# Attention and two MLPs on one core: batch 1's gate and value tiles computed as products of 2x2 blocks

## The chip, the cores and the metric

The kernel is one program on one core of a Trainium2 chip. The metric is the time of the program on the device in microseconds; the median of the runs counts. TensorE (PE in the rows) multiplies, ScalarE (ACT) and VectorE (DVE) read its results from the eight PSUM banks, GpSimd (POOL) works in SBUF, and SyncE (SP) issues DMAs. Each engine works through its own queue in order, and semaphores are all that ties one queue to another.

## The reference

Windowed attention with block summaries (batch 2, 8 heads, 768 tokens, width 64) gives x of 1536 tokens by 512. Two MLPs follow, and the change touches only the first, and of that only batch 1:

```
rms = sqrt(mean(x*x) + 1e-6);  xn = x / rms * rms_g
g   = xn @ w_gate              # 512 x 1536
val = xn @ w_val               # 512 x 1536
y   = (g * sigmoid(g) * val) @ w_out      # 1536 x 512
h   = y @ w_in                 # 512 x 2048
out = (h - tanh(h)) @ w_out2   # 2048 x 512
```

## The kernel before

Every fp32 matrix is held as two fp32r parts, high (a rounded copy, made by ScalarE) and low (the remainder, a subtraction on VectorE), and each product of fp32 matrices is three matmuls: high by high, high by low, low by high. Inputs of the MLPs lie transposed: `xT_hi[g]` and `xT_lo[g]` hold batch g's x^T as 4 chunks of 128 rows by 768 tokens. Tokens are worked in halves of 384 (NB), so that a result fits a bank.

The order of the work is written out by hand for each engine. Batch 0's attention comes first; batch 1's attention is woven into batch 0's first MLP. Then come batch 0's projection down (`down_first`, tiles z), batch 0's second MLP, batch 1's first MLP (gates and values, then `down_first`), and batch 1's second MLP.

In the first MLP the 1536 columns of `w_gate` and `w_val` make 12 row tiles j of 128 (J1). For each j and token half b, `gate` and `val` make 4 chunks x 3 = 12 matmuls each (through `project`) into banks `XB` and `YB`. ScalarE takes the tanh, VectorE makes `sg` and `pd` (`gated`, `product`), ScalarE makes the high part of h and VectorE the low part (`low_h`). Tiles of weights come by DMA into `x_raw` (gate) and `y_raw` (value), two slots each, are split into `x_hi`, `x_lo`, `y_hi`, `y_lo`, and are used for two halves.

The second MLP already multiplies by seven instead of eight (Winograd's form of Strassen's scheme). A pair p of row tiles and the two token halves make a 2x2 block matrix; `quarter` is one block product, 2 chunks x 3 = 6 matmuls of 128 x 384. GpSimd makes sums of the weights' blocks (`add_weights`: four adds of 128x256 into `ws_raw`), which ScalarE and VectorE split. Sums accumulate in one bank, and ScalarE keeps the intermediate states (`keep_part`). Between the quarters of pair p stand the 12 output units (`down_unit`, 3 matmuls of 128 x 512) of pair p-1. That covers the waits between quarters. In the trace the second MLP's tiles `h2_hi` and `h2_lo` are named `h_hi` and `h_lo`.

## Time and profile before

| | us |
|---|---|
| median of 3 runs (645.47 to 649.68) | 645.63 |
| the profiled execution, as a run | 643.8 |
| its span, first to last instruction | 642.1 |
| TensorE busy | 625.2 (97%) |
| VectorE busy | 386.6 (60%) |
| ScalarE busy | 293.8 (46%) |
| GpSimd busy | 122.5 (19%) |

The span is divided by the order of work. By first instructions on TensorE, batch 0's second MLP ends at 362.59 us, batch 1's gates and values at 462.45 us, and its projection down at 512.37 us. Matmuls are pipelined, so that the time that one costs is the distance from its start to the next one's start, not its printed duration. The granted TensorE clock is 1.00 in every stretch, which is the higher of its two levels, 2.4 GHz.

### The profile page before, as it was taken

To read this page: it belongs to the slowest core of one execution; us is meant where nothing else is said; L and a number is where in the kernel's file an instruction comes from. 1 tells how busy PE (TensorE), PEld (TensorE's weight loads), DVE (VectorE), ACT (ScalarE), POOL (GpSimd) and SP (SyncE) were. 2 spreads that over 40 slices of the span, in tenths; PEclk is the share of its full clock that TensorE was granted. 3 is DMA by queue.
4 is the path that set the end of the run, shared out by engine and by line. 5 is a ranking of instruction groups with operands and counts; after the bars stand their busy time and mean duration, and the time that the engine had idled before them with its cause. 6 is when DMAs were issued, how large, how long until landed. Compare 5 with 4: busy or idle time off the path is not lost.

```text
span 642.1 us, 10665 instructions
## 1 busy us (share of the span) xinstructions
PE 625.2 (97%) x4086; PEld 583.5 (91%) x4086; DVE 386.6 (60%) x647; ACT 293.8 (46%) x564; POOL 122.5 (19%) x175
## 2 busy tenths in 40 slices
PE   8888999999999999999999999999999999999997
PEld 7567889999999998988899899999999989998886
DVE  3787667666653569766664455555433398666643
ACT  4685454454533347555554333333233275555532
POOL 3674612021210222222220000000100033222200
PEclk9999999999999999999999999999999999999999
DMA  9994913321412123222212422111313013222102
GB/s 260 211 207 126 200 50 91 91 58 34 102 40 74 51 91 84 80 66 67 65 50 66 148 66 63 53 54 47 99 50 114 2 51 99 76 71 66 35 1 98
DMA packets 96170, 53.91 MB, mean 84 GB/s; under 512 B 33720, under 2 KB 90296, under 8 KB 95928
## 3 DMA queue, kind: packets, MB, share of 16 engines
q1 hardware_dynamic: 94824, 50.87, 30.7%
q10 hardware_dynamic: 1296, 2.36, 1.0%
q8 instruction: 33, 0.54, 0.4%
q14 instruction: 17, 0.14, 0.1%
HBM read 50.07 MB, written 3.15 MB: 83 GB/s over the span
## 4 chain that ended last, share of the span: by engine, by line
PE 87%; SPq 5%; ACT 3%; DVE 3%; issue 1%; DMA 1%; POOL 0%; DVEq 0%; POOLq 0%; ACTq 0%
PE bank L726 14%; PE bank L728 14%; PE bank L727 14%; PE bank L834 7%; PE bank L833 7%; PE bank L832 7%; PE bank L786 6%; PE bank L788 6%; PE bank L790 6%; SPq L384 3%; PE bank L710 1%; PE bank L586 1%; PE bank L690 1%; PE bank L661 1%; ACT kT L1010 1%
## 5 line engine op out<-in xcount | busy, mean ns | idle before, releaser
L1412 DVE TENSOR_TENSOR h_lo<-pd,h_hi 128x384 fp32r<-128x384 f32 x112 | 67.2, 601 | 38.9 <-ACT h_hi L1090 24.5
L834 PE MATMUL bank<-y_hi,h_lo 128*128 128x512 f32 x192 | 75.5, 393 | 0.0
L833 PE MATMUL bank<-y_lo,h_hi 128*128 128x512 f32 x192 | 75.4, 393 | 0.0
L832 PE MATMUL bank<-y_hi,h_hi 128*128 128x512 f32 x192 | 75.3, 392 | 0.0
L572 POOL TENSOR_TENSOR ws_raw<-x_raw 128x256 f32<-128x256 f32 x16 | 12.2, 760 | 325.4 <-DMA x_raw<-in_moe_w_in_dram 146.3
L726 PE MATMUL bank<-xT_hi,x_hi 128*128 128x384 f32 x192 | 65.1, 339 | 1.4 <-DVE xT_lo L1408 1.4
L726 PE MATMUL bank<-xT_hi,y_hi 128*128 128x384 f32 x192 | 65.7, 342 | 0.0
L726 PE MATMUL bank<-h_hi,z_hi 128*128 128x384 f32 x192 | 64.9, 338 | 0.0
L728 PE MATMUL bank<-h_hi,z_lo 128*128 128x384 f32 x192 | 64.5, 336 | 0.0
L727 PE MATMUL bank<-h_lo,z_hi 128*128 128x384 f32 x192 | 64.5, 336 | 0.0
L728 PE MATMUL bank<-xT_hi,y_lo 128*128 128x384 f32 x192 | 64.3, 335 | 0.0
L728 PE MATMUL bank<-xT_hi,x_lo 128*128 128x384 f32 x192 | 64.2, 335 | 0.0
L727 PE MATMUL bank<-xT_lo,y_hi 128*128 128x384 f32 x192 | 64.2, 334 | 0.0
L727 PE MATMUL bank<-xT_lo,x_hi 128*128 128x384 f32 x192 | 64.2, 334 | 0.0
L1090 ACT CAST h_hi<-pd 128x384 fp32r<-128x384 f32 x48 | 24.7, 514 | 85.8 <-DVE pd L1440 85.7
L1440 DVE SCALAR_TENSOR_TENSOR pd<-sg,bank 128x384 f32<-128x384 f32 x48 | 26.6, 553 | 39.3 <-PE bank L728 38.9
L1493 DVE TENSOR_TENSOR total<-part,bank 128x384 f32<-128x384 f32 x48 | 26.4, 553 | 34.8 <-ACT part L1123 28.9
L1123 ACT COPY part<-bank 128x384 f32<-128x384 f32 x48 | 23.0, 479 | 52.0 <-PE bank L790 50.8
L834 PEld LDWEIGHTS bank<-y_hi,h_lo 128*128 128x128 f32 x192 | 36.0, 188 | 8.2
L1412 DVE TENSOR_TENSOR y_lo<-y_raw,y_hi 128x512 fp32r<-128x512 f32 x56 | 40.2, 722 | 0.1
L833 PEld LDWEIGHTS bank<-y_lo,h_hi 128*128 128x128 f32 x192 | 36.0, 188 | 4.0
L1133 ACT ACTIVATE th<-total 128x384 f32<-128x384 f32 x48 | 25.2, 525 | 31.5 <-DVE total L1493 31.5
(141 smaller groups left out, 1457.3 us busy)
## 6 DMA issues: line engine op xcount, KB each, us to landing
x_raw<-in_moe_w_in_dram SPq DMA_DIRECT2D x32, 256.0 KB, 3.3
y_raw<-in_moe_w_out_dram SPq DMA_DIRECT2D x32, 256.0 KB, 2.7
x_raw<-in_moe_w_gate_dram SPq DMA_DIRECT2D x24, 256.0 KB, 3.2
y_raw<-in_moe_w_val_dram SPq DMA_DIRECT2D x24, 256.0 KB, 3.3
z_raw<-in_moe_w_out_dram SPq DMA_DIRECT2D x16, 384.0 KB, 3.4
k_rows<-in_k_dram SPq DMA_DIRECT2D x8, 384.0 KB, 6.1
qn<-in_q_dram SPq DMA_DIRECT2D x12, 256.0 KB, 6.7
vw_early<-in_v_dram SPq DMA_DIRECT2D x12, 192.0 KB, 6.1
```

Of the source, the lines that this page charges most:

```text
L726: nc.tensor.matmul(dst, w_hi, a_hi, start=start, stop=False)
L727: nc.tensor.matmul(dst, w_hi, a_lo, start=False, stop=False)
L728: return nc.tensor.matmul(dst, w_lo, a_hi, start=False, stop=stop)
L786: nc.tensor.matmul(dst, w_hi[:, r, :], a_hi[:, r, :], start=start and r == 0, stop=False, skip_group_check=True)
L788: nc.tensor.matmul(dst, w_hi[:, r, :], a_lo[:, r, :], start=False, stop=False, skip_group_check=True)
L790: last = nc.tensor.matmul(dst, w_lo[:, r, :], a_hi[:, r, :], start=False, stop=r == 1, skip_group_check=True)
L832: nc.tensor.matmul(AB[t][:], a_hi, w_hi, start=begins, stop=False, skip_group_check=True)
L833: nc.tensor.matmul(AB[t][:], a_hi, w_lo, start=False, stop=False, skip_group_check=True)
L834: last = nc.tensor.matmul(AB[t][:], a_lo, w_hi, start=False, stop=ends, skip_group_check=True)
L1412: nc.vector.tensor_tensor(dst, full, high.bitcast(f32), ALU.subtract).then_inc(done, 1)
L1440: nc.vector.scalar_tensor_tensor(out=pd[:, s, :], in0=sg[:, s, :], scalar=0.5, in1=YB[vpos % 2][:, 0:NB], op0=ALU.mult, op1=ALU.mult).then ...
L1493: nc.vector.tensor_tensor(total[:, TOTALS.index(name[:3]), :], kept, accumulator, ALU.add).then_inc(total_done, 1)
```

## The change

- Batch 1's gates and values are made pair by pair (6 pairs i of row tiles, 2i and 2i+1) by the same scheme of seven block products. Each is done for gate and value in turn (`up_pair` in all engines): P1, P2, P5, P6, P7, P4, P3, 14 `quarter` calls of 6 matmuls for a pair. Before, a pair was 8 calls of `project` with 12 matmuls.
- Nothing stands between the quarters of a pair on TensorE. P2 accumulates on a copy of P1 that ScalarE writes into another bank (`keep_up`). P6, P7 and P4 accumulate on P1 in place, with copies of the state after P6 (`kept2`) and P7 (`kept3`). VectorE joins P5 to them, one join directly into the bank in which P3 then accumulates.
- GpSimd forms the sums of the weights' blocks in eight adds of 128x256 per pair (`add_up_weights`), for the next pair while TensorE works on this one. ScalarE and VectorE split them (`us_hi`, `us_lo`; 1024 elements for the gates, the same for the values, which ScalarE does in two instructions of 512). The second row tile of a pair is split only in its lower half (256 elements).
- The sums of batch 1's x^T (`x_sums`) are formed during pairs 1 to 7 of batch 0's second MLP: 14 VectorE instructions of 128x768, two in each pair, and 4 ScalarE copies of 128x768. They stand behind the pair's `split_sums`.
- At the end of batch 0 the six output stores move from ScalarE's queue to SP's, which issues them behind the loads of the second pair of gate and value tiles. ScalarE and VectorE split the first sums between their copies of output rows. The first two z tiles of batch 1 are split in the last pair of gates and values, and no longer in batch 0.

The diff, cut to the products, the sums and the orders of the engines:

```diff
+        UP_ORDER = [(name, m) for name in ("P1", "P2", "P5", "P6", "P7", "P4", "P3") for m in (GATE, VAL)]
+        UP_TILES = ("C11", "C22", "C21", "C12")
+        KEPT = [("P1", GATE), ("P1", VAL), ("P6", GATE), ("P6", VAL), ("P7", GATE), ("P7", VAL)]
...
+            def add_up_weights(i):
+                if i < 2:
+                    pool.wait_ge(quarter_mm, PRODUCTS * NP)
+                else:
+                    pool.wait_ge(block_mm, len(UP_ORDER) * (i - 1))
+                for m in (GATE, VAL):
+                    raw, landed, at = (x_raw, x_in, 8 * i) if m == GATE else (y_raw, y_in, 8 * i + 4)
+                    for row in range(2):
+                        pool.wait_ge(landed[row], (up_weight(i, row) - row) * 8 + 16)
+                    s = [us_raw[i % 2][:, m, k, :, :] for k in range(4)]
+                    a11, a12, a21, a22 = (raw[:, row, c:c + KH, :] for row in range(2) for c in (0, KH))
+                    nc.gpsimd.tensor_tensor(s[S1], a21, a22, ALU.add).then_inc(us_added, 1)
+                    nc.gpsimd.tensor_tensor(s[S3], a11, a21, ALU.subtract).then_inc(us_added, 1)
+                    pool.wait_ge(us_added, at + 1)
+                    nc.gpsimd.tensor_tensor(s[S2], s[S1], a11, ALU.subtract).then_inc(us_added, 1)
+                    pool.wait_ge(us_added, at + 3)
+                    nc.gpsimd.tensor_tensor(s[S4], a12, s[S2], ALU.subtract).then_inc(us_added, 1)
...
+                return {"P1": lambda: weights(0, top) + x(top, first),
+                        "P2": lambda: weights(0, bottom) + x(bottom, first),
+                        "P3": lambda: sums(S4) + x(bottom, rest),
+                        "P4": lambda: weights(1, bottom) + x_sums(T4),
+                        "P5": lambda: sums(S1) + x(top, rest),
+                        "P6": lambda: sums(S2) + x_sums(T2),
+                        "P7": lambda: sums(S3) + x_sums(T3)}[name]()
+            def up_pair(i):
+                def product(name, m, dst, start=False):
+                    quarter(dst, *up_operands(i, name, m), start=start).then_inc(block_mm, 1)
+                if i == 0:
+                    pe.wait_ge(ts_dve, 14)
+                for m in (GATE, VAL):
+                    pe.wait_ge(y_lo_done if m else x_lo_done, up_weight(i, 0) + 1)
+                    if i:
+                        pe.wait_ge(c22_done, 2 * (i - 1) + m + 1)
+                    elif m:
+                        pe.wait_ge(out_act, 1)
+                    product("P1", m, sum_bank(i, m), start=True)
+                for m in (GATE, VAL):
+                    pe.wait_ge(kept_done, kept_no(i, "P1", m))
+                    product("P2", m, c11_bank(m))
+                for m in (GATE, VAL):
+                    pe.wait_ge(us_lo_done, 2 * i + m + 1)
+                    if i:
+                        pe.wait_ge(prod_done if m else x_bank_free, up_pos(i - 1, "C21") + 1)
+                    elif m:
+                        pe.wait_ge(out_dve, 1)
+                    product("P5", m, p5_bank(i, m), start=True)
+                for m in (GATE, VAL):
+                    product("P6", m, sum_bank(i, m))
+                for m in (GATE, VAL):
+                    pe.wait_ge(kept_done, kept_no(i, "P6", m))
+                    product("P7", m, sum_bank(i, m))
+                for m in (GATE, VAL):
+                    pe.wait_ge(y_lo_done if m else x_lo_done, up_weight(i, 1) + 1)
+                    pe.wait_ge(kept_done, kept_no(i, "P7", m))
+                    product("P4", m, sum_bank(i, m))
+                for m in (GATE, VAL):
+                    pe.wait_ge(joined, 2 * i + m + 1)
+                    product("P3", m, c12_bank(m))
...
+            def split_up_sums(i, m, part=slice(0, 4)):
+                act.wait_ge(us_added, 8 * i + 4 * m + 4 if part.stop == 4 else 8 * i + 4 * m + 3)
+                nc.scalar.copy(us_hi[i % 2][:, m, part, :, :], us_raw[i % 2][:, m, part, :, :]).then_inc(us_hi_done, 1)
...
+            def up_pair(i):
+                if i:
+                    tanh_up(i - 1, "C12")
+                    high_up(i - 1, "C21")
+                keep_up(i, "P1", GATE)
+                if i + 1 < J1 // 2:
+                    split_x(up_weight(i + 1, 0))
+                keep_up(i, "P1", VAL)
+                if i:
+                    high_up(i - 1, "C12")
+                tanh_up(i, "C11")
+                if i + 1 < J1 // 2:
+                    split_y(up_weight(i + 1, 0))
+                    split_x(up_weight(i + 1, 1))
+                    split_y(up_weight(i + 1, 1))
+                else:
+                    split_z(ZG)
+                    split_z(ZG + 1)
+                if i + 1 < J1 // 2:
+                    split_up_sums(i + 1, GATE)
+                    split_up_sums(i + 1, VAL, slice(S1, S3))
+                high_up(i, "C11")
+                keep_up(i, "P6", GATE)
+                if i + 1 < J1 // 2:
+                    split_up_sums(i + 1, VAL, slice(S3, 4))
+                keep_up(i, "P6", VAL)
+                keep_up(i, "P7", GATE)
+                keep_up(i, "P7", VAL)
+                tanh_up(i, "C22")
+                tanh_up(i, "C21")
+                high_up(i, "C22")
...
+            def x_sums(i):
+                hi11, hi21 = (xT_hi[1][:, c:c + KH, 0:NB].bitcast(f32) for c in (0, KH))
+                lo11, lo21 = (xT_lo[1][:, c:c + KH, 0:NB].bitcast(f32) for c in (0, KH))
+                hi12, hi22 = (xT_hi[1][:, c:c + KH, NB:S].bitcast(f32) for c in (0, KH))
+                lo12, lo22 = (xT_lo[1][:, c:c + KH, NB:S].bitcast(f32) for c in (0, KH))
+                t1 = kT[1][:, 0:KH, NB:S]
+                t2, t3, t4 = (ts_raw[:, k, :, :] for k in (T2, T3, T4))
+                dve.wait_ge(ts_dve, 2 * (i - 1))
+                if i == 1:
+                    dve.wait_ge(z_mm, ZG)
+                    dve.wait_ge(xT_lo_done, NT)
+                    nc.vector.tensor_tensor(ts_raw_hi[:, T3, :, :], hi22, hi12, ALU.subtract).then_inc(ts_dve, 1)
+                    nc.vector.tensor_tensor(t3, lo22, lo12, ALU.subtract).then_inc(ts_dve, 1)
...
+                if i == 4:
+                    nc.vector.tensor_tensor(t1, t2, t4, ALU.add).then_inc(ts_dve, 1)
+                    dve.wait_ge(ts_dve, 7)
+                    nc.vector.tensor_tensor(t2, hi22, t1, ALU.subtract).then_inc(ts_dve, 1)
+                if i == 5:
+                    nc.vector.tensor_tensor(t2, t2, lo22, ALU.add).then_inc(ts_dve, 1)
+                    dve.wait_ge(ts_act, 2)
+                    low(xT_lo[1][:, 0:KH, NB:S], t1, xT_hi[1][:, 0:KH, NB:S], ts_dve)
...
+            def join(i, m):
+                dve.wait_ge(kept_done, kept_no(i, "P6", m))
+                dve.wait_ge(block_mm, block_no(i, "P5", m))
+                if i:
+                    dve.wait_ge(prod_done if m else x_bank_free, up_pos(i - 1, "C12") + 1)
+                else:
+                    dve.wait_ge(out_dve, 2 + m)
+                nc.vector.tensor_tensor(c12_bank(m), kept2[:, m, :], p5_bank(i, m), ALU.add).then_inc(joined, 1)
+            def join_c22(i, m):
+                dve.wait_ge(kept_done, kept_no(i, "P7", m))
+                nc.vector.tensor_tensor(kept3[:, m, :], kept3[:, m, :], p5_bank(i, m), ALU.add).then_inc(c22_done, 1)
...
+            def up_pair(i):
+                last = i + 1 == J1 // 2
+                if i:
+                    gated_up(i - 1, "C12")
+                    low_up(i - 1, "C21")
+                    product_up(i - 1, "C12")
+                if not last:
+                    split_x(up_weight(i + 1, 0))
+                if i:
+                    low_up(i - 1, "C12")
+                if not last:
+                    split_y(up_weight(i + 1, 0))
+                gated_up(i, "C11")
+                if not last:
+                    split_x(up_weight(i + 1, 1))
+                product_up(i, "C11")
+                if not last:
+                    split_y(up_weight(i + 1, 1))
+                else:
+                    split_z(ZG)
+                    split_z(ZG + 1)
+                low_up(i, "C11")
+                if not last:
+                    split_up_sums(i + 1, GATE)
+                join(i, GATE)
+                join(i, VAL)
+                join_c22(i, GATE)
+                join_c22(i, VAL)
+                gated_up(i, "C22")
+                product_up(i, "C22")
+                gated_up(i, "C21")
+                low_up(i, "C22")
+                product_up(i, "C21")
+                if not last:
+                    split_up_sums(i + 1, VAL)
```

What stands on an engine now, at three places. GpSimd, batch 0's last weight sums and what follows them; before, these rows go straight to batch 1's second MLP:

```order
L572 TENSOR_TENSOR ws_raw0<-x_raw 128x256
L573 TENSOR_TENSOR ws_raw0<-x_raw 128x256
L575 TENSOR_TENSOR ws_raw0<-ws_raw0,x_raw 128x256
L577 TENSOR_TENSOR ws_raw0<-x_raw,ws_raw0 128x256
L572 TENSOR_TENSOR ws_raw1<-x_raw 128x256
```

Of the change, in its place, a part of the 48 new adds, with numbers left off the buffers:

```order
L717 TENSOR_TENSOR us_raw<-x_raw,us_raw 128x256
L712 TENSOR_TENSOR us_raw<-y_raw 128x256
L713 TENSOR_TENSOR us_raw<-y_raw 128x256
L715 TENSOR_TENSOR us_raw<-us_raw,y_raw 128x256
L717 TENSOR_TENSOR us_raw<-y_raw,us_raw 128x256
L694 TENSOR_TENSOR ws_raw<-x_raw 128x256
```

The adds for six pairs, eight for each, now stand ahead of batch 1's `ws_raw` adds.

ScalarE, batch 1's gates and values, before (two row tiles' rows repeat like this):

```order
L1066 CAST x_hi<-x_raw 128x512
L1073 CAST y_hi<-y_raw 128x512
L1085 ACTIVATE th<-bank 128x384
L1090 CAST h_hi<-pd 128x384
L1085 ACTIVATE th<-bank 128x384
L1090 CAST h_hi<-pd 128x384
```

and now, a pair from its first tanh to its last copy of the state:

```order
L1338 ACTIVATE th<-bank 128x384
L1274 CAST y_hi2<-y_raw 128x512
L1266 CAST x_hi2<-x_raw 128x256
L1274 CAST y_hi2<-y_raw 128x256
L1310 CAST us_hi1<-us_raw1 128x1024
L1310 CAST us_hi1<-us_raw1 128x512
L1291 CAST h_hi<-pd 128x384
L1329 COPY kept2<-bank 128x384
L1310 CAST us_hi1<-us_raw1 128x512
L1329 COPY kept2<-bank 128x384
L1329 COPY kept3<-bank 128x384 x2
```

The copies of the next pair's sums, which wait for GpSimd, now stand ahead of this pair's copy of P6, for which TensorE waits before P7.

VectorE, a pair of batch 0's second MLP, before:

```order
L1412 TENSOR_TENSOR h2_lo<-pd,h2_hi 128x384
L1412 TENSOR_TENSOR ws_lo1<-ws_raw1,ws_hi1 128x1024
L1493 TENSOR_TENSOR total<-part,bank 128x384
L1502 TENSOR_TENSOR pd<-total,th 128x384
L1502 TENSOR_TENSOR pd<-bank,th 128x384
```

and now:

```order
L1697 TENSOR_TENSOR h2_lo<-pd,h2_hi 128x384
L1697 TENSOR_TENSOR ws_lo0<-ws_raw0,ws_hi0 128x1024
L1697 TENSOR_TENSOR ts_lo<-ts_raw,ts_hi 128x768
L1758 TENSOR_TENSOR ts_raw<-xT_lo1 128x768
L1892 TENSOR_TENSOR total<-part,bank 128x384
L1901 TENSOR_TENSOR pd<-total,th 128x384
```

Two instructions of 768 elements stand between the split of the weight sums and the total that the pair needs next.

## Rows read from the trace of the kernel before

**Rows 1.** The page: span, busy time of the engines, and the chain by engine.

```profile
span 642.1 us, 10665 instructions
...
PE 625.2 (97%) x4086; PEld 583.5 (91%) x4086; DVE 386.6 (60%) x647; ACT 293.8 (46%) x564; POOL 122.5 (19%) x175
...
PE 87%; SPq 5%; ACT 3%; DVE 3%; issue 1%; DMA 1%; POOL 0%; DVEq 0%; POOLq 0%; ACTq 0%
```

**Rows 2.** Busy time by stretch: window, length, PE, PEld, DVE, ACT, POOL, clock, DMA.

```profile
362.59:462.50 99.91, 99.91 (x578) 99.91 (x577) 52.97 (x93) 34.59 (x70) 3.17 (x4) 1.00 0.25 74
```

**Rows 3.** TensorE in order of time (start, us): first instructions of two stretches.

```profile
362.59 0.34 PE L726 MATMUL bank<-xT_hi,x_hi 128*128 128x384 f32 x1
...
462.45 0.33 PE L726 MATMUL bank<-h_hi,z_hi 128*128 128x384 f32 x1
```

**Rows 4.** All engines in order of time, first pair of batch 1's second MLP.

```profile
512.37 0.34 PE L786 MATMUL bank<-xT_hi,x_hi 128*128 128x384 f32 x1
...
515.88 0.34 PE L790 MATMUL bank<-tq_hi,ws_lo 128*128 128x384 f32 x1
...
516.25 0.48 ACT L1123 COPY part<-bank 128x384 f32<-128x384 f32 x1 [0.94 <-PE bank L790]
...
516.40 0.34 PE L790 MATMUL bank<-xT_hi,x_lo 128*128 128x384 f32 x1
...
516.88 0.42 PE L786 MATMUL bank<-tq_hi,ws_hi 128*128 128x384 f32 x1
```

**Rows 5.** VectorE and GpSimd in order of time, a pair of batch 0's second MLP.

```profile
321.08 0.55 DVE L1412 TENSOR_TENSOR h_lo<-pd,h_hi 128x384 fp32r<-128x384 f32 x1
...
321.98 0.74 POOL L572 TENSOR_TENSOR ws_raw<-x_raw 128x256 f32<-128x256 f32 x1 [12.11 <-PE bank L790]
...
322.39 0.75 DVE L1412 TENSOR_TENSOR h_lo<-pd,h_hi 128x384 fp32r<-128x384 f32 x1
...
322.68 1.05 POOL L573 TENSOR_TENSOR ws_raw<-x_raw 128x256 f32<-128x256 f32 x1
...
323.06 1.09 DVE L1502 TENSOR_TENSOR pd<-total,th 128x384 f32<-128x384 f32 x1
...
323.69 1.05 POOL L575 TENSOR_TENSOR ws_raw<-ws_raw,x_raw 128x256 f32<-128x256 f32 x1
...
324.82 0.74 POOL L577 TENSOR_TENSOR ws_raw<-x_raw,ws_raw 128x256 f32<-128x256 f32 x1
```

**Rows 6.** One tile's instructions, `ws_raw`: minimum, median and maximum in ns.

```profile
L573 POOL TENSOR_TENSOR ws_raw<-x_raw x16: 742/1052/1191, 217.8 to 598.7; 128x256 f32<-128x256 f32 x16
L575 POOL TENSOR_TENSOR ws_raw<-ws_raw,x_raw x16: 733/1055/1451, 218.9 to 599.7; 128x256 f32<-128x256 f32 x16
```

**Rows 7.** Groups by line and shape, 362 to 640 us (busy, mean ns | idle before).

```profile
L1412 DVE TENSOR_TENSOR ws_lo<-ws_raw,ws_hi 128x1024 fp32r<-128x1024 f32 x8 | 9.8, 1226 | 4.4 <-ACT ws_hi L1119 4.4
...
L1412 DVE TENSOR_TENSOR z_lo<-z_raw,z_hi 128x768 fp32r<-128x768 f32 x6 | 5.7, 958 | 10.1 <-ACT z_hi L1080 10.1
```

**Rows 8.** VectorE in order of time, a pair of batch 0's second MLP.

```profile
328.42 0.69 DVE L1412 TENSOR_TENSOR y_lo<-y_raw,y_hi 128x512 fp32r<-128x512 f32 x1
...
329.02 0.42 DVE L1412 TENSOR_TENSOR x_lo<-x_raw,x_hi 128x256 fp32r<-128x256 f32 x1
...
330.61 1.22 DVE L1412 TENSOR_TENSOR ws_lo<-ws_raw,ws_hi 128x1024 fp32r<-128x1024 f32 x1 [0.71 <-ACT ws_hi L1119]
...
333.86 0.56 DVE L1493 TENSOR_TENSOR total<-part,bank 128x384 f32<-128x384 f32 x1 [2.02 <-ACT part L1123]
```

**Rows 9.** ScalarE in order of time, batch 0's second MLP.

```profile
329.15 0.48 ACT L1123 COPY part<-bank 128x384 f32<-128x384 f32 x1
...
329.53 1.05 ACT L1119 CAST ws_hi<-ws_raw 128x1024 fp32r<-128x1024 f32 x1
...
333.35 0.48 ACT L1123 COPY part<-bank 128x384 f32<-128x384 f32 x1 [2.76 <-PE bank L790]
...
340.31 0.52 ACT L1139 CAST h_hi<-pd 128x384 fp32r<-128x384 f32 x1
...
340.72 0.62 ACT L1073 CAST y_hi<-y_raw 128x512 fp32r<-128x512 f32 x1
```

More of the change, by code:

```diff
@@ L238, in halves, with blocks @@
             return [(j, 0), (j, 1), (j + 1, 0), (j + 1, 1)]
+        def blocks(i):
+            return [(2 * i, 0), (2 * i + 1, 1), (2 * i + 1, 0), (2 * i, 1)]
         first_order = {(g, j, b): n for g in range(G)
-                       for n, (j, b) in enumerate(h for i in range(J1 // 2) for h in halves(g, i))}
+                       for n, (j, b) in enumerate(h for i in range(J1 // 2) for h in (blocks(i) if g else halves(g, i)))}
         def first_pos(g, j, b):
@@ L422, in _ @@
                 if g:
-                    for j in range(J1):
-                        load_xy(weight_no(g, j))
+                    for i in range(J1 // 2):
+                        for row in range(2):
+                            load_x(up_weight(i, row))
+                        for row in range(2):
+                            load_y(up_weight(i, row))
+                        if i == 1:
+                            for t in range(TT):
+                                sp.wait_ge(out_dve if t % 2 else out_act, t // 2 + 1)
+                                sp.dma_start(out_v[:, t, :], stage[:, t, :]).then_inc(out_sent, 16)
+                    for m in range(2):
+                        load_z(ZG * g + m)
                 load_pair(g * NP)
-                for m in range(2, ZG + 2 if g + 1 < G else ZG):
+                for m in range(2, ZG):
                     load_z(ZG * g + m)
@@ L816, in operands, with up_operands, weights, sums @@
                         "P7": lambda: sums(S3) + x2_sums(T3)}[name]()
+            def up_operands(i, name, m):
+                top, bottom, first, rest = slice(0, KH), slice(KH, KC), slice(0, NB), slice(NB, S)
+                w_hi, w_lo = (t[2 * (i % 2)] for t in ((xw_hi, xw_lo) if m == GATE else (yw_hi, yw_lo)))
+                def weights(row, half):
+                    return w_hi[:, row, half, :], w_lo[:, row, half, :]
+                def sums(k):
+                    return us_hi[i % 2][:, m, k, :, :], us_lo[i % 2][:, m, k, :, :]
+                def x(half, tokens):
+                    return xT_hi[1][:, half, tokens], xT_lo[1][:, half, tokens]
+                def x_sums(k):
+                    return ts_hi[:, k, :, :], ts_lo[:, k, :, :]
+                return {"P1": lambda: weights(0, top) + x(top, first),
[5 more added lines that the diff above has]
+                        "P7": lambda: sums(S3) + x_sums(T3)}[name]()
@@ L995, in _ @@
                     for i in range(J1 // 2):
-                        for j, b in halves(g, i):
-                            gate(g, j, b)
-                            val(g, j, b)
+                        up_pair(i)
                     for d in range(KC):
@@ new lines, in split_up_sums @@
+            def split_up_sums(i, m):
+                dve.wait_ge(us_hi_done, 3 * i + 2 * m + 1)
+                low(us_lo[i % 2][:, m, :, :, :], us_raw[i % 2][:, m, :, :, :], us_hi[i % 2][:, m, :, :, :], us_lo_done)
+            def join(i, m):
+                dve.wait_ge(kept_done, kept_no(i, "P6", m))
+                dve.wait_ge(block_mm, block_no(i, "P5", m))
+                if i:
+                    dve.wait_ge(prod_done if m else x_bank_free, up_pos(i - 1, "C12") + 1)
+                else:
+                    dve.wait_ge(out_dve, 2 + m)
+                nc.vector.tensor_tensor(c12_bank(m), kept2[:, m, :], p5_bank(i, m), ALU.add).then_inc(joined, 1)
```

290 lines of the change are left out of this document (230 added, 60 removed).

## The prediction

> **What bounds the kernel now.** I read the page first. TensorE is busy 97% of the span, and 87% of the chain that ended last is TensorE's own work [rows 1]. The reader should see that nothing else carries a share, so a removed matmul is worth its own time, if nothing else comes late in its place. Next I read the stretch that the change rewrites, by its window. TensorE never pauses in it, while VectorE works 52.97 us of 99.91, ScalarE 34.59 and GpSimd 3.17, all at clock 1.00 [rows 2]. The stretch runs from 362.59 to 462.45 us [rows 3] and holds 12 row tiles x 2 halves x 2 (gate, value) x 12 = 576 matmuls, so one costs 99.86 / 576 = 0.1734 us. The printed 0.34 us overlaps with the next one. Third, I looked for a place where quarters stand on TensorE with nothing between them, as all of them will in this stretch: the first pair of batch 1's second MLP [rows 4]. Last, I looked at what VectorE and GpSimd do to each other when both work [rows 5], since both are loaded much more.
>
> **What is removed.** Six pairs x 14 quarters x 6 matmuls = 504 take the place of 576. The order of the changed program has 72 fewer TensorE rows, so the saving in number is sure. In price, 504 x 0.1734 = 87.4 us at the rate of the old stretch. Among quarters the rate is a little lower: from 512.37 to 516.40 stand 24 matmuls, 23 distances, 0.175 each [rows 4]. That place is the nearer one, so I take 504 x 0.175 = 88.2, a gain of 99.9 - 88.2 = 11.7 us before any wait, and 12.5 as the best case. A pair then takes TensorE 14.7 us, a quarter 1.05.
>
> **What each engine has to do in 14.7 us.** From start to start, VectorE takes 0.60 for 512 elements [rows 8]. By the same gap of 0.09 under the printed time, it takes 0.47 for 384, 0.33 for 256 and 1.14 for 1024 [rows 5, 7, 8]. A pair has 16 instructions of 384 (four each of sg, pd and low parts, four joins), two of 512, two of 256 and two of 1024: 7.5 + 1.2 + 0.7 + 2.3 = 11.7 us. ScalarE takes 0.41 for a cast or tanh of 384, 0.38 for a copy out of a bank, and by the same gap of 0.1 it takes 0.52 for 512 [rows 9]. Eight, six and four of these (512 elements, twice for weights and twice for sums), two of 256 (0.3) and one of 1024 (0.95) make 9.2 us. GpSimd has eight adds, 0.74 each at best and 0.70 from start to start [rows 5]: 5.7 us. Each fits, VectorE by the least, so the question is the order and not the sum.
>
> **Copies between quarters.** P2 waits for ScalarE's copy of P1, P7 for that of P6, P4 for that of P7. The price of this wait stands in the trace. P6's last matmul starts at 515.88, the copy at 516.25, and P7, which waits for it, at 516.88, 1.00 us after [rows 4]. In the change one quarter of the other matrix stands between, so the next matmul is due 7 x 0.175 = 1.22 us after. The wait is covered by 0.2 us, if ScalarE is free at that moment. The copy of P1 goes from bank to bank, and the join writes a bank; no row shows either. I take the 0.48 of the copy out of a bank [rows 9], since the source is the same. At 0.3 us more it would cost 0.1 us for each of six pairs, 0.6 in all. It could also be shorter, which gains nothing, as TensorE then is not waiting. The Trainium skill ("ScalarE: Activation LUTs", Step-by-step: what each stage is for) says that ScalarE's way to PSUM is faster than its way to SBUF; no row here shows it, and by it this term is nil.
>
> **Where ScalarE isn't free.** It handles P6's copy only behind the first 512 elements of the next pair's value sums and the high part of C11. Those sums wait for GpSimd's seventh add, and GpSimd begins when the pair before has ended, 0.2 us into the pair. So the chain that I expect to decide is: seven adds, then 0.03 + 0.52 (split) + 0.41 (high part) + 0.48 (copy) + 0.15 to TensorE = 1.6 us (0.03 and 0.15 are the gaps ahead of 516.25 and behind 516.73 [rows 4]). P7 is due at 8 x 1.05 = 8.4 us. The seventh add must therefore be done 6.8 us into the pair.
>
> Alone, seven adds take 7 x 0.70 and 0.2 for waits on one another, and end at 5.3. At the pace of a pair of the second MLP it is four adds in 3.55 and three more in 2.76 (323.69 + 1.05 - 321.98), which ends at 6.5 [rows 5]: still in time. But in that pair only two of four adds met VectorE, and each then took 1.05 in place of 0.74. What happens there is seen in the four ends. The low part that starts at 322.39 ends 0.42 after the first add's end; the second add ends 0.59 after that; VectorE's `pd` of 323.06 ends 0.42 after that, and the third add 0.59 after that. They take turns, as if one waited for the other's end. This holds for VectorE's instructions with two inputs in SBUF. In the first 7 us of a pair VectorE will have six such: the rest of a split of 1024 (0.5), two low parts (0.42 each) and splits of 512, 512 and 256 (0.56, 0.56, 0.29), 2.7 us together. Laid out in order, some 2.2 of it falls in front of an add. The seventh add then ends at 5.3 + 2.2 = 7.5, and P7 starts at 9.1 instead of 8.4. That is **0.75 us for each of pairs 1 to 4**, 3.0 us. The ends are 0 (adds at the pace of the rows) and 1.2 (all 2.7 in front) for each pair. Pair 0 escapes, since the adds for its successor can begin before batch 0's output is done, and pair 5 has no successor.
>
> The Trainium skill ("SBUF — State Buffer", Who interferes with whom) has a rule that speaks against this change. A VectorE instruction with two SBUF inputs and a GpSimd instruction that reads SBUF share a read interface, and the second to come is blocked until the first ends. By that rule, the trace agrees, with 1.05 for 0.74 and 1.09 for 0.55. Without the rule the sum would be 11.7 us gained, with it 8.7.
>
> **The sums of x^T.** 14 VectorE instructions of 768 elements at 0.96, 0.87 from start to start [rows 7], two in each of seven pairs: 1.8 us. They stand where VectorE ends at 331.83 and then waits 2.02 us for the kept P7, until 333.86 [rows 8]. They fit with 0.2 to spare, and I cost them at nothing. If that cover is gone, the total comes late; some 1.7 us of quarters and units still stand before P3 needs it. No `ws_raw` add runs at that time (the four end by 325.6 [rows 5]). ScalarE's four copies of 768, 0.84 each (halfway between 0.62 for 512 and 1.05 for 1024 [rows 9]), start when VectorE's first sum is done, near 332.8, and move the copy at 333.35 by 0.3 us. P4 is due two units later, so this is free too. The upper bound is 0.5 us in each pair, 3 us. The output stores leave ScalarE's queue; on SP's they stand ahead of the loads of pair 2, which nobody needs for 14 us. The z tiles are loaded at pair 5's start, into a place of their own, and are split 4 to 6 us into it, before P6's copy at 7.4.
>
> **The sum.** 99.9 - 88.2 - 3.0 = 8.7 us. The profiled execution took 643.8 with a span of 642.1; it becomes 635.1 with 633.4. The median of the runs stands 1.8 above the profiled one, and becomes 645.6 - 8.7 = **636.9 us**.
>
> **Rivals.**
> (a) No wait at all: GpSimd keeps the pace of the rows. The stretch is 87.4 to 88.2, the time 633.1 to 633.9. For it speaks that every engine has room; against it, VectorE at 80% instead of 53% of the stretch. Chance 0.25.
> (b) The forecast, 635.5 to 638.5. Chance 0.45.
> (c) VectorE becomes the bound. If each of the eight adds also holds VectorE up for 0.59, its 11.7 become 16.4 us, more than TensorE's 14.7, and six pairs take 98.4: 645.6 - 1.5 = 644.1. For it, `pd` at 323.06 took 1.09 in place of 0.55; against it, over half of VectorE's instructions have an input in a bank, and the second half of a pair is free of adds. Anything between (b) and this, with late batch 0 sums (up to 3 us), belongs here: 638.5 to 644.5. Chance 0.24.
> (d) Slower than before: GpSimd's chain alone. The slowest add in the trace took 1.45 [rows 6]. If all did, the seventh ends 0.2 + 10.2 = 10.4 us in, P7 starts at 12.0, 3.6 us late, and with 2.5 in pair 0 the stretch is 88.2 + 16.9 = 105.1: 650.9. It decides from 11.7 us of waits in all, 2.6 for each of the four and 1.5 in pair 0, which is a mean add of 1.3 us. Chance 0.04.
> (e) The change doesn't do what it says, for instance because a weight sum or a kept state makes TensorE wait in every quarter, with the same result as (d). Chance 0.02.
>
> **How the numbers follow.** A measurement of this kernel tells 1%, 6.5 us, from no change; that border is 639.2. (a), (b) and a third of (c) lie below: 0.78. The rest of (c) is within 1%: 0.16. Beyond 652.1 only the end of (d) and (e) lie; I leave 0.06 for them and for what I don't see. The range reaches from (a)'s lower end, 633.0, into (c), to 642.0.
>
> **What would show it.** The stretch has 504 matmuls at 0.173 to 0.176 us apart. Four waits before P7, in pairs 1 to 4, are ended by ScalarE's copy into `kept2`, of some 0.75 us. Adds of `us_raw` mean 0.9 to 1.1 us. ScalarE's second cast of `us_hi` (512) is released by GpSimd. In batch 0's second MLP TensorE doesn't pause, as before. The prediction is wrong if adds stay near 0.85 (then (a)), if TensorE waits for `us_lo`, `joined` or P1's copy, or if VectorE has no idle time left in a pair.

## The result: 635.9 us after 645.6, and the profile after

The changed kernel takes 635.88 us (median of 4 runs, 634.96 to 637.34) against 645.55 (4 runs), a ratio of 0.9845 with a 95% interval of 0.981 to 0.9881, so 1.2 to 1.9% faster. The forecast was 636.9, range 633.0 to 642.0.

The page's head and the window of the rewritten stretch, the rows that answer to [rows 1] and [rows 2] (the window's columns are length, PE, PEld, DVE, ACT, POOL, clock, DMA share, GB/s):

```profile
span 634.1 us, 10771 instructions
...
PE 615.5 (97%) x4014; PEld 571.9 (90%) x4014; DVE 425.3 (67%) x697; ACT 322.7 (51%) x622; POOL 170.2 (27%) x223
```

```profile
363.58:454.45 90.87, 88.50 (x506) 87.22 (x504) 75.33 (x127) 58.67 (x121) 38.56 (x39) 1.00 0.33 98
```

The stretch took 99.86 us [rows 3] and now takes 90.87, from TensorE's first matmul on `x_hi` at 363.58 to its first on `h_hi` and `z_hi` at 454.45. TensorE is now idle in 2.4 of these us by the profile, VectorE is busy for 75.3 of 90.9 us instead of 53.0 of 99.9, and GpSimd for 38.6 instead of 3.2. What stands behind the stretch lasts 179.65 us in both kernels (642.1 - 462.45 and 634.1 - 454.45). The stretch begins 0.99 us later. So the span's 8.0 us are 8.99 from the stretch, less 0.99 in front of it.

TensorE's waits, longest in total first:

```profile
PE bank L927 <- ACT kept L1329: 2.4, 4, 0.6
```

Four waits, at one place. TensorE in order of time around the first of them, in pair 1, which begins at 378.17:

```profile
378.17 0.33 PE L927 MATMUL bank<-xT_hi,x_hi 128*128 128x384 f32 x1
...
386.32 0.34 PE L931 MATMUL bank<-ts_hi,us_lo 128*128 128x384 f32 x1
387.24 0.44 PE L927 MATMUL bank<-ts_hi,us_hi 128*128 128x384 f32 x1 [0.59 <-ACT kept L1329]
387.52 0.34 PE L929 MATMUL bank<-ts_lo,us_hi 128*128 128x384 f32 x1
387.69 0.34 PE L931 MATMUL bank<-ts_hi,us_lo 128*128 128x384 f32 x1
```

P7 was due 0.17 after 386.32 and starts 0.92 after it, 0.75 late. The distance to the next matmul is 0.28 instead of 0.17, so that a wait costs some 0.85 in all. The others, at 402.68, 418.12 and 433.54, are alike: 4 x 0.85 = 3.4 us. The rest of the stretch, 90.87 - 3.4 = 87.5, is 504 matmuls at 0.1735. The chain that ends in the wait, GpSimd's adds first (start, us):

```profile
378.41 1.26 POOL L712 TENSOR_TENSOR us_raw<-x_raw 128x256 f32<-128x256 f32 x1 [8.10 <-PE bank L931]
379.63 1.05 POOL L713 TENSOR_TENSOR us_raw<-x_raw 128x256 f32<-128x256 f32 x1
380.64 1.18 POOL L715 TENSOR_TENSOR us_raw<-us_raw,x_raw 128x256 f32<-128x256 f32 x1
381.90 0.94 POOL L717 TENSOR_TENSOR us_raw<-x_raw,us_raw 128x256 f32<-128x256 f32 x1
382.80 1.19 POOL L712 TENSOR_TENSOR us_raw<-y_raw 128x256 f32<-128x256 f32 x1
383.95 0.92 POOL L713 TENSOR_TENSOR us_raw<-y_raw 128x256 f32<-128x256 f32 x1
384.83 0.92 POOL L715 TENSOR_TENSOR us_raw<-us_raw,y_raw 128x256 f32<-128x256 f32 x1
385.82 0.74 POOL L717 TENSOR_TENSOR us_raw<-y_raw,us_raw 128x256 f32<-128x256 f32 x1
```

and ScalarE, in the same pair:

```profile
383.00 1.05 ACT L1310 CAST us_hi<-us_raw 128x1024 fp32r<-128x1024 f32 x1
385.78 0.62 ACT L1310 CAST us_hi<-us_raw 128x512 fp32r<-128x512 f32 x1 [1.73 <-POOL us_raw L715]
386.30 0.51 ACT L1291 CAST h_hi<-pd 128x384 fp32r<-128x384 f32 x1
386.72 0.47 ACT L1329 COPY kept<-bank 128x384 f32<-128x384 f32 x1
```

The seventh add ends at 385.75, 7.6 us into the pair. ScalarE has waited 1.73 us for it, casts (385.78), makes the high part of C11 (386.30) and copies P6 (386.72, until 387.19), and P7 starts. Only the eighth add takes 0.74 us; the others take 0.92 to 1.26.

In batch 0's second MLP two short waits are new. VectorE in pair 1, with the two instructions for the sums of x^T ahead of the total, and ScalarE in pair 2, with the cast ahead of the copy of P7:

```profile
256.90 0.95 DVE L1750 TENSOR_TENSOR ts_raw_hi<-xT_hi 128x768 f32<-128x768 f32 x1
257.77 0.95 DVE L1751 TENSOR_TENSOR ts_raw<-xT_lo 128x768 f32<-128x768 f32 x1
258.64 0.55 DVE L1892 TENSOR_TENSOR total<-part,bank 128x384 f32<-128x384 f32 x1
```

```profile
271.36 0.84 ACT L1297 CAST ts_hi<-ts_raw 128x768 fp32r<-128x768 f32 x1 [2.16 <-DVE ts_raw L1753]
272.10 0.47 ACT L1407 COPY part<-bank 128x384 f32<-128x384 f32 x1
```

TensorE starts P3 at 259.24, right behind the total and 0.16 late, and P4 at 272.72, behind the copy and 0.13 late. With the longer distances that follow, they cost 0.26 and 0.21 us. These 0.47 are half of the 0.99 by which the stretch begins later. The other half is there at 183.75 us already (183.22 before), ahead of everything that was changed except the buffers' places. It isn't the change's: the kernel e4_drop72 below is the kernel before up to this stretch, and reaches it at 363.60. In the profiles below it begins anywhere from 363.58 to 366.87 (and at 368.33 in e3_one_more_add's, whose first 100 us had a mean granted clock of 0.95), so the front of the kernel varies by itself.

### The profile page after: what moved, and what is told of

Its sections match the earlier page's. It is cut to its first block, busy times and chain, and to the rows that moved or that the text cites. A ratio compares the mean times of both kernels' runs of the same rounds, so it can differ in the third digit from the quotient of the medians.

```text
span 634.1 us, 10771 instructions
## 1 busy us (share of the span) xinstructions
PE 615.5 (97%) x4014; PEld 571.9 (90%) x4014; DVE 425.3 (67%) x697; ACT 322.7 (51%) x622; POOL 170.2 (27%) x223
## 4 chain that ended last, share of the span: by engine, by line
PE 81%; POOL 5%; SPq 5%; ACT 4%; DVE 3%; issue 1%; DMA 1%; DVEq 0%; POOLq 0%; ACTq 0%
PE bank L870 9%; PE bank L927 9%; PE bank L871 9%; PE bank L872 9%; PE bank L929 9%; PE bank L931 9%; PE bank L1036 7%; PE bank L1035 7%; PE bank L1034 7%; SPq L497 3%; POOL us_raw L712 2%; PE bank L730 2%; PE bank L854 1%; POOL us_raw L715 1%; POOL us_raw L713 1%
## 5 line engine op out<-in xcount | busy, mean ns | idle before, releaser
L1697 DVE TENSOR_TENSOR h_lo<-pd,h_hi 128x384 fp32r<-128x384 f32 x112 | 70.3, 629 | 34.6 <-ACT h_hi L1291 18.9
L1034 PE MATMUL bank<-y_hi,h_hi 128*128 128x512 f32 x192 | 75.3, 392 | 0.0
L1291 ACT CAST h_hi<-pd 128x384 fp32r<-128x384 f32 x48 | 24.6, 513 | 38.8 <-DVE pd L1727 32.3
L1697 DVE TENSOR_TENSOR y_lo<-y_raw,y_hi 128x512 fp32r<-128x512 f32 (+1 forms) x56 | 40.4, 726 | 2.2 <-ACT y_hi L1274 2.1
L1901 DVE TENSOR_TENSOR pd<-total,th 128x384 f32<-128x384 f32 x48 | 33.5, 697 | 9.6 <-ACT th L1417 8.9
L1034 PEld LDWEIGHTS bank<-y_hi,h_hi 128*128 128x128 f32 x192 | 36.0, 187 | 4.0
L1423 ACT CAST h_hi<-pd 128x384 fp32r<-128x384 f32 x64 | 32.6, 512 | 12.7 <-DVE pd L1901 12.6
L606 POOL TENSOR_TENSOR sm<-sm,mx 128x480 f32<-128x480 f32 x24 | 23.7, 986 | 49.6 <-DVE mx L1666 49.6
L870 PEld LDWEIGHTS bank<-h_hi,z_hi 128*128 128x128 f32 x192 | 36.1, 188 | 0.2 <-issue 0.2
L871 PEld LDWEIGHTS bank<-h_lo,z_hi 128*128 128x128 f32 x192 | 36.1, 188 | 0.0
L872 PEld LDWEIGHTS bank<-h_hi,z_lo 128*128 128x128 f32 x192 | 36.1, 188 | 0.0
```

The lines of the kernel that those rows point to most:

```text
L870: nc.tensor.matmul(dst, w_hi, a_hi, start=start, stop=False)
L871: nc.tensor.matmul(dst, w_hi, a_lo, start=False, stop=False)
L872: return nc.tensor.matmul(dst, w_lo, a_hi, start=False, stop=stop)
L1034: nc.tensor.matmul(AB[t][:], a_hi, w_hi, start=begins, stop=False, skip_group_check=True)
L1423: nc.scalar.copy(h2_hi[:, p % NP % 2, row, b, :], pd[:, no % 2, :]).then_inc(h2_hi_done, 1)
L1697: nc.vector.tensor_tensor(dst, full, high.bitcast(f32), ALU.subtract).then_inc(done, 1)
```

## The experiments

Times are medians of each kernel's runs, ratios against runs of the kernel before in the same round of measurements. There were four rounds: the changed kernel; e1 to e4; e5 to e7; e8. The kernel before took 645.55, 645.14, 645.86 and 646.11 us in them. The stretch is from TensorE's first matmul of the gates to its first of the projection down, in the profile.

| kernel | us | ratio and 95% interval | stretch, us |
|---|---|---|---|
| before | 645.6 | | 99.86 |
| changed | 635.88 | 0.9845 (0.981 to 0.9881) | 90.87 |
| e1_order | 632.43 | 0.9809 (0.9781 to 0.9837) | 87.39 |
| e2_port | 633.28 | 0.982 (0.9788 to 0.9852) | 87.38 |
| e3_one_more_add | 640.8 | 0.9936 (0.9915 to 0.9956) | 94.90 |
| e4_drop72 | 632.5 | 0.9801 (0.9771 to 0.9832) | 87.38 |
| e5_order_and_sums | 633.43 | 0.9793 (0.9761 to 0.9826) | 87.38 |
| e6_late_cast_one_more | 635.32 | 0.9823 (0.9786 to 0.986) | 89.51 |
| e7_order_again | 632.96 | 0.9787 (0.9759 to 0.9816) | 87.39 |
| e8_product_first | 633.98 | 0.9811 (0.9783 to 0.984) | 88.58 |

What stands behind the stretch is 179.59 to 179.69 us in every one of them, so that all differences are in the stretch or ahead of it.

**ScalarE's order (e1_order).** In ScalarE's `up_pair`:

```diff
                 if i + 1 < J1 // 2:
                     split_up_sums(i + 1, GATE)
-                    split_up_sums(i + 1, VAL, slice(S1, S3))
                 high_up(i, "C11")
                 keep_up(i, "P6", GATE)
+                if i + 1 < J1 // 2:
+                    split_up_sums(i + 1, VAL, slice(S1, S3))
+                keep_up(i, "P6", VAL)
                 if i + 1 < J1 // 2:
                     split_up_sums(i + 1, VAL, slice(S3, 4))
-                keep_up(i, "P6", VAL)
```

> Only ScalarE's order in a gate and value pair is changed: the two casts of the next pair's value sums (512 elements each) stand behind the copies of P6 (gate) and P6 (value), no longer ahead of the first. Theory (the wait before P7 comes from ScalarE standing behind GpSimd's seventh add): the four waits before P7 vanish, 0.85 us each with the longer second distance, and the stretch falls from 90.9 to 87.4 us, the time by 3.4 us to some 632.5. Rival 1 (the copy of P6 is late for another reason, as ScalarE's load): the waits stay at 0.5 us or more. Rival 2 (the wait only moves): TensorE waits as long before P5 of the next pair for the low parts of the value sums, or before P3 for the join, and the time stays within 1 us of 635.9.

The stretch's window, and ScalarE in a pair:

```profile
363.82:451.21 87.39, 87.39 (x506) 87.39 (x505) 79.75 (x127) 59.85 (x121) 39.90 (x39) 1.00 0.34 102
```

```profile
385.01 0.51 ACT L1291 CAST h_hi<-pd 128x384 fp32r<-128x384 f32 x1 [0.72 <-DVE pd L1812]
385.88 0.48 ACT L1329 COPY kept<-bank 128x384 f32<-128x384 f32 x1 [0.36 <-PE bank L931]
386.26 0.62 ACT L1310 CAST us_hi<-us_raw 128x512 fp32r<-128x512 f32 x1
```

TensorE is busy in all 87.39 us. The copy of P6 (385.88) now waits for nothing but P6, and the cast follows it. 90.87 - 87.39 = 3.48 us, the four waits. They went nowhere else: neither rival holds. The adds are no faster here: in pairs 1 to 4 their mean is 1.05 to 1.09 us, and in pair 1 the seventh ends at 385.99, 7.6 us into the pair, as in the changed kernel. So the order alone removed the waits. The 95% intervals of the two ratios overlap (0.9781 to 0.9837 and 0.981 to 0.9881); that the edit gains 3.5 us rests on the stretch.

The margin shrinks from pair to pair, though. VectorE's product of C11 starts 6.02 us into pair 1 and 6.11, 6.20 and 6.30 into pairs 2, 3 and 4, so TensorE doesn't wait within six pairs; more pairs weren't tried.

**The price of 72 matmuls alone (e4_drop72).** In the kernel before:

```diff
-                for c in range(KC):
+                n_c = KH if g and b and s else KC
+                for c in range(n_c):
                     last = three(dst, w_hi[:, s, c, :], w_lo[:, s, c, :], xT_hi[g][:, c, tokens],
-                                 xT_lo[g][:, c, tokens], c == 0, c == KC - 1)
+                                 xT_lo[g][:, c, tokens], c == 0, c == n_c - 1)
```

> The kernel before with 72 matmuls left out and nothing else changed: batch 1's gates and values of the odd row tiles use only two of the four chunks for the second token half. It is the price of the 72 matmuls alone. Theory (TensorE bounds the stretch by the number of its matmuls, 0.1734 us each): 12.5 us less than before, 633.1, and the stretch 87.4 us. Rival (part of a removed matmul's time comes back, as the stretch is not purely TensorE's): less than 11 us. The distance from there to the changed kernel's 635.9 is what the scheme costs elsewhere: 3.4 us of waits and up to 1 us in batch 0.

The stretch is 87.38, 12.48 us less for 72 matmuls, 0.1733 each, and the time 632.5. The kernel of e1_order makes the same number of matmuls in the same 87.4 us, with VectorE, ScalarE and GpSimd far busier (79.8, 59.9 and 39.9 us in the window above, against 51.5, 34.0 and 3.1 in the window of the same stretch here). So the block scheme, put in this order, costs TensorE nothing in the stretch.

**Are the adds slow by VectorE (e2_port)?** VectorE's splits for pairs 1 to 5 (`other` is a bank's content; `split_y` is changed alike, and the joins also wait for these splits, so that the bank isn't written before they have read it):

```diff
+            def low_from_bank(dst, full, c, done):
+                width = (c.stop - c.start) * P
+                other = bank[5][:, 0:width].rearrange("p (c n) -> p c n", n=P)
+                nc.vector.tensor_tensor(dst, full, other, ALU.subtract).then_inc(done, 1)
...
-                low(xw_lo[place(n)][:, s, c, :], x_raw[:, s, c, :], xw_hi[place(n)][:, s, c, :], x_lo_done)
+                if STEPS + 2 <= n < STEPS + J1:
+                    low_from_bank(xw_lo[place(n)][:, s, c, :], x_raw[:, s, c, :], c, x_lo_done)
```

> In the changed kernel, VectorE's four splits of the next pair's weights (512, 512, 256, 256 elements) subtract the content of a PSUM bank in place of the high part, so that they have one input in SBUF and not two; sizes, order and waits stay. The low parts of batch 1's gate and value weights of pairs 1 to 5 are therefore not the remainders. Theory (VectorE's instructions with two SBUF inputs and GpSimd's adds take turns): the adds that met these splits fall back towards 0.74 us, the seventh add ends some 1.5 us earlier in the pair, the waits before P7 vanish, and the time is near 632.5. Rival (the adds are slow by themselves, by their operands or by DMA traffic): the eight adds of a pair keep their durations (mean near 1.03) and the waits of 0.6 to 0.75 us stay, 635.9.

GpSimd and VectorE in one pair:

```profile
393.48 1.25 POOL L712 TENSOR_TENSOR us_raw<-x_raw 128x256 f32<-128x256 f32 x1 [7.54 <-PE bank L931]
394.69 1.06 POOL L713 TENSOR_TENSOR us_raw<-x_raw 128x256 f32<-128x256 f32 x1
395.70 0.74 POOL L715 TENSOR_TENSOR us_raw<-us_raw,x_raw 128x256 f32<-128x256 f32 x1
396.52 1.07 POOL L717 TENSOR_TENSOR us_raw<-x_raw,us_raw 128x256 f32<-128x256 f32 x1
397.55 0.74 POOL L712 TENSOR_TENSOR us_raw<-y_raw 128x256 f32<-128x256 f32 x1
398.26 0.73 POOL L713 TENSOR_TENSOR us_raw<-y_raw 128x256 f32<-128x256 f32 x1
398.96 0.73 POOL L715 TENSOR_TENSOR us_raw<-us_raw,y_raw 128x256 f32<-128x256 f32 x1
```

```profile
392.92 1.22 DVE L1697 TENSOR_TENSOR us_lo<-us_raw,us_hi 128x1024 fp32r<-128x1024 f32 x1
...
394.52 0.63 DVE L1697 TENSOR_TENSOR h_lo<-pd,h_hi 128x384 fp32r<-128x384 f32 x1
...
395.53 0.68 DVE L1702 TENSOR_TENSOR x_lo<-x_raw,bank 128x512 fp32r<-128x512 f32 x1
396.44 0.56 DVE L1697 TENSOR_TENSOR h_lo<-pd,h_hi 128x384 fp32r<-128x384 f32 x1 [0.23 <-ACT h_hi L1291]
397.58 0.69 DVE L1702 TENSOR_TENSOR y_lo<-y_raw,bank 128x512 fp32r<-128x512 f32 x1 [0.59 <-ACT y_hi L1274]
```

Only a second input moved from SBUF to a bank. The three adds that still take more than 0.74 us overlap what still has two SBUF inputs: the rest of the split of 1024 and the low parts of h at 394.52 and 396.44. Those beside the changed splits (395.53 and 397.58) take 0.74, and the splits take 0.68 and 0.69, where they took 0.83 and 0.87 in the mean in the changed kernel:

```profile
L1697 DVE TENSOR_TENSOR y_lo<-y_raw,y_hi 128x512 fp32r<-128x512 f32 x5 | 4.4, 874 | 2.1 <-ACT y_hi L1274 2.1
L1697 DVE TENSOR_TENSOR x_lo<-x_raw,x_hi 128x512 fp32r<-128x512 f32 x5 | 4.1, 829 | 0.0
```

GpSimd's busy time in the stretch falls from 38.6 to 33.1 us, at nearly the same DMA share (0.34, and 0.33 in the changed kernel). The seventh add ends at 399.69, 6.2 us behind the first one's start, against 7.3 in the changed kernel, and TensorE doesn't wait: the theory holds, the rival (slow by themselves or by DMA traffic) falls. The seventh add came 1.1 us earlier where I had expected 1.5.

**One more add (e3_one_more_add).** The diff, in `add_up_weights`:

```diff
+                    if m == VAL:
+                        nc.gpsimd.tensor_tensor(s[S4], a21, a22, ALU.add).then_inc(one_more, 1)
                     nc.gpsimd.tensor_tensor(s[S1], a21, a22, ALU.add).then_inc(us_added, 1)
```

> The changed kernel with one more add of 128x256 on GpSimd for each pair, ahead of the value sums (its output is overwritten; nothing is left out). Theory (TensorE's wait follows the seventh add one for one): each of the four waits grows by the length of an add, 0.7 to 1.2 us, and pair 0 gets a wait too; the time rises by 4 x 0.9 to 5 x 0.9, 3.5 to 5 us, to some 640. Rival (ScalarE's or VectorE's load sets the wait, GpSimd has slack): less than 1 us more.

TensorE's waits, and the second of them:

```profile
PE bank L932 <- ACT kept L1334: 6.1, 5, 1.3
```

```profile
393.89 0.44 PE L932 MATMUL bank<-ts_hi,us_hi 128*128 128x384 f32 x1 [1.28 <-ACT kept L1334]
```

Five waits now, pair 0's among them. In this pair the add that ScalarE waits for ends at 392.41, 8.0 us behind the first one's start at 384.38; in the changed kernel it was 7.3 (385.75 - 378.41), so it comes 0.69 us later. P7 starts 1.44 us late, in place of 0.75, which is 0.69 more: the wait follows the add one for one. The stretch grows by 4.03 us, 4 x 0.7 + 1.2 for pair 0, at a granted clock of 1.00. VectorE's product of C11 starts 6.03 us into this pair, as in the changed kernel (6.02), so that here the ninth add doesn't hold it up.

**The sums of x^T (e5_order_and_sums, e7_order_again).** Both have the order of e1_order; e5 also moves `x_sums` in pair 1 behind `add_total(p, "C22", ...)`, and in pair 2 `x_sums_high` behind the copy of P7:

```diff
-                if g + 1 < G:
+                if g + 1 < G and i > 1:
                     x_sums(i)
                 add_total(p, "C22", "P5", 3 * p + 3, part[:, 2, :], VB)
+                if g + 1 < G and i == 1:
+                    x_sums(i)
```

> The kernel with ScalarE's casts of the value sums behind the copies of P6, and two more moves in batch 0's second MLP: in pair 1 VectorE's two instructions for the sums of x^T stand behind the total C22, and in pair 2 ScalarE's cast of them stands behind the copy of P7. Theory (the two waits of 0.26 and 0.21 us that the changed kernel shows there are these instructions, ahead of a total and of a copy for which TensorE waits): both waits go, and the time is 0.5 us under that of the kernel with the new order alone, 632.0, which the trace can show and the times hardly. Rival (the waits come from the GpSimd and VectorE meeting in pair 1): they stay.

> The kernel with the new order of ScalarE alone, once more on the same chip as the two kernels beside it, so that they can be compared: 632.4, no wait before P7, and the waits of 0.2 to 0.3 us in pairs 1 and 2 of batch 0's second MLP.

In the trace of e5 both waits are gone. In e7's, P3 at 260.15 and P4 at 273.62 are 0.20 and 0.14 late, as in the changed kernel. So the instructions' place was the cause. The times don't show it (633.43 and 632.96, on one chip), as the spread from the front of the kernel is larger than 0.5 us. I take e1_order's edit as the better version, 632.4 and 633.0 us in two measurements, some 3 us under the changed kernel by the medians, with a stretch of 87.39 us in both.

**One more add, with the casts late (e6_late_cast_one_more, e8_product_first).** In e6 ScalarE's casts of the value sums stand behind the copy of P7 (value), with the extra add of e3. In e8, additionally, on VectorE:

```diff
                 gated_up(i, "C11")
-                if not last:
-                    split_x(up_weight(i + 1, 1))
                 product_up(i, "C11")
+                if not last:
+                    split_x(up_weight(i + 1, 1))
                 if not last:
                     split_y(up_weight(i + 1, 1))
```

> The changed kernel with one more add on GpSimd per pair (nothing left out), and both casts of the value sums behind the last copy (P7, value) of the pair. Theory (it is the place of the casts in ScalarE's queue, not GpSimd's load, that makes TensorE wait): the 1.44 us waits before P7 are gone in spite of the extra add, and the time is within 0.7 us of the kernel with the new order, 632.4. Rival (GpSimd's load costs by itself): 635 or more, with TensorE waiting before P5 for the low parts of the value sums.

This one missed: 2.1 us more in the stretch than e1_order, and 2.9 or 2.4 in the time (against its two measurements), where I had said at most 0.7. The time is the rival's, 635 or more, but the place isn't: TensorE waits 0.4 us (0.5 with the next distance) before P7 in pairs 1 to 4, and not before P5. ScalarE from the end of pair 0 into pair 1, which begins at 378.63, then VectorE:

```profile
375.04 1.14 ACT L1315 CAST us_hi<-us_raw 128x512 fp32r<-128x512 f32 x2
376.08 0.53 ACT L1343 ACTIVATE th<-kept 128x384 f32<-128x384 f32 x1
...
386.41 0.51 ACT L1296 CAST h_hi<-pd 128x384 fp32r<-128x384 f32 x1 [1.21 <-DVE pd L1816]
386.82 0.85 ACT L1334 COPY kept<-bank 128x384 f32<-128x384 f32 x2
```

```profile
376.64 0.56 DVE L1804 SCALAR_TENSOR_TENSOR sg<-th,kept 128x384 f32<-128x384 f32 x1 [0.90 <-ACT th L1343]
...
379.31 1.38 DVE L1702 TENSOR_TENSOR us_lo<-us_raw,us_hi 128x1024 fp32r<-128x1024 f32 x1
...
382.79 1.09 DVE L1702 TENSOR_TENSOR h_lo<-pd,h_hi 128x384 fp32r<-128x384 f32 x1
383.80 1.23 DVE L1702 TENSOR_TENSOR y_lo<-y_raw,y_hi 128x512 fp32r<-128x512 f32 x1
...
385.83 0.54 DVE L1816 SCALAR_TENSOR_TENSOR pd<-sg,bank 128x384 f32<-128x384 f32 x1
```

The high part of C11 at 386.41 waited 1.21 us for VectorE's product (385.83), and not for GpSimd. The product starts 7.20 us into the pair, where it was 6.02 in the changed kernel and in e1_order. Of these 1.18 us, 1.0 is there when the pair begins: the split of the value sums starts 0.68 into the pair, against 0.31 ahead of it in the changed kernel:

```profile
377.86 1.22 DVE L1697 TENSOR_TENSOR us_lo<-us_raw,us_hi 128x1024 fp32r<-128x1024 f32 x1
```

That comes from the edit itself. The two casts of the value sums (375.04) now stand ahead of the tanh of C22, which starts 12.04 us into pair 0 and not 11.00 as in the changed kernel, and VectorE waited 0.90 us for it (376.64). The longer low part and split (1.09 and 1.23 us, where 0.55 and 0.69 are usual) add only the last 0.2. The ninth add isn't needed for it: e3 has it too, and its product starts at 6.03; and in pair 0 of e6, with nine adds but no late casts before it, TensorE doesn't wait. So it is again the place of the casts, behind the last copy but ahead of a tanh that VectorE needs. No run has these late casts with eight adds, so that this split of the cause is read from traces and not tested.

> As the kernel with one more add and the late casts, with VectorE's product of C11 ahead of its split of 256 elements (x, second row tile) and no longer behind it. In the kernel without this move ScalarE's high part of C11 waited for that product, then came the copy of P6, and TensorE waited 0.4 us before P7 in pairs 1 to 4 (0.5 with the longer second distance). Theory (the other direction of the same turn-taking: GpSimd's adds hold VectorE up, whose product is now the last thing before the copy): the product starts 0.4 us earlier, the waits shrink to 0.1 us or nothing, and the stretch goes from 89.5 to 87.4 to 87.9 us. Rival (the product is held by something that also holds it when it stands first, as the tanh of C11): the waits stay at 0.3 us or more and the stretch near 89.5.

The waits before P7 are 0.1 to 0.2 us (0.2 to 0.3 with the next distance), the stretch 88.58. It falls by 0.93, where I had expected 1.6 to 2.1. The rival (0.3 us or more, near 89.5) falls: the copy's lateness follows the product. But it starts only 0.2 to 0.3 us earlier (6.90 to 7.01 us into pairs 1 to 4, after 7.20), since `sg` of C11 ahead of it is as late as in e6 (6.32 to 6.44, after 6.32; 5.14 in the changed kernel). The casts ahead of the tanh of C22 are still there, and what the theory named, adds that hold VectorE up, isn't the main part of the delay.

## Why the prediction was right, point by point

- **The number of matmuls and their worth: right, and a size off.** The 72 matmuls are worth 12.48 us (e4_drop72), the best case of the forecast. I had taken 0.175 us for a matmul among quarters from [rows 4], for 11.7 us. In the new stretch they stand 0.1735 apart, as in the old one. That term was 0.8 us too dear for the stretch. What makes 0.175 in [rows 4] stays open; it isn't the quarters, since 504 matmuls in quarters run at 0.1734 in e1_order.
- **The copies between quarters: right.** P2 and P4 never wait, and P7 only where ScalarE comes late. The copy from bank to bank took 0.46 us, against 0.48 into SBUF, within the 0.2 us of cover.
- **ScalarE behind the seventh add: right in place, number and size.** Said: the seventh add 7.5 us into a pair, P7 0.75 late in pairs 1 to 4. Measured: 7.6 us, 0.75, pairs 1 to 4, none in pair 0 or 5. Undone by order with the adds as slow as before (e1), by relief of the adds (e2), and answered one for one by an add more (e3). That 0.75 is met to the digit is luck: the prediction's own 9.1 - 8.4 is 0.7, the link from the seventh add's end to P7 took 1.49 (387.24 - 385.75) and not 1.6, and P7 was due at 8.32. The term was 0.4 us too small, since a wait also lengthens the distance behind it by 0.10; I had read the start times in [rows 4] without looking at the next distance.
- **Turns between VectorE and GpSimd: right, and shown.** They were read in one pair [rows 5]. The adds' mean in pairs 1 to 4 is 1.03 us (0.9 to 1.1 said), and seven of them take 7.3 us, 2.2 more than the 5.1 that the prediction gave them alone, which is the delay that it worked out. e2_port changes only where an input lies, and the adds beside it fall to 0.74. The rule of the Trainium skill ("SBUF — State Buffer", Who interferes with whom), that a VectorE instruction with two SBUF inputs and a GpSimd instruction reading SBUF block each other, agrees with this run. The other direction, adds that hold VectorE up, shows in the low part at 382.79 in e6, which took 1.09 us.
- **The sums of x^T: near nil, not nil.** The term was 0 with an upper bound of 3 us (0.5 in each of seven pairs would be 3.5); it is 0.47. I had read the cover in one pair of the steady part [rows 8] and held it for all. Pair 1, the first, had less. There VectorE's split of the weight sums ends late, and the two instructions are 0.9 us longer than the one of z that they replace. In pair 2 the cast moved the copy of P7 by 0.7 us (from 270.61 in the kernel before to 272.10, less the 0.78 by which everything is later there), and I had worked out 0.3 in another pair.
- **The sum.** For the span: said 8.7, of which the stretch all. Measured 8.0: stretch 8.99 (12.48 - 3.48, rounded), batch 0 -0.47, front -0.52. That the stretch came out within 0.3 us of the forecast is in part luck: the errors of rate and of wait, 0.8 and 0.4 to 0.5, have opposite signs. The medians differ by 9.7, 1.7 more than the spans of the two profiled executions; the beginning of the stretch varies by more than that between profiles.
- **Rivals.** (a), no wait, is what the kernel becomes with e1_order: 632.4, just under its 633.1 to 633.9. (c), VectorE as the bound, didn't come: it is busy for 75.3 of 90.9 us. In e6 it is the last before the copy, but mostly through ScalarE's casts and not through the adds. (d) has its slope confirmed by e3: at 0.69 us per added add, some 3 more adds in each pair would be needed to lose the gain of 9 us (an estimate: 9 / (5 x 0.69) = 2.6).

## What to carry to other kernels

When a scheme moves work from the bounding engine to three others, add up their loads, but decide by order: find the instruction that the bounding engine waits for, and look whether an instruction that waits for a slower engine stands ahead of it in its queue, for work that is needed only later. One swap in such a queue was worth 3.5 of the 12.5 us here. Then look at what the moved instruction stands ahead of in its new place: one step too far back (e6), it delayed a tanh, the tanh delayed VectorE, and TensorE waited again. Price an instruction of two SBUF inputs beside GpSimd adds with turns in it, and a slack that you read in one iteration separately for the first ones.
